# Reordering the first passes of a fused attention and MLP kernel: maxima, gate factors, weight loads and the first finished x

## The reference

```python
# attention: B=4, H=8, S=576, D=64
scores = scale * q @ k^T, causal mask
a = exp(scores - rowmax); a /= a.sum(-1) + 1e-9
local = a @ v
q_p = phi(q)                       # phi(x) = (x if x > 0 else exp(x) - 1) + 1
mem_out = (q_p @ M_prev) / (q_p . z_prev + 1e-6)
g = 1 / (1 + exp(-beta))
x = g * mem_out + (1 - g) * local  # -> 2304 tokens x 512
# MLP 1 (512 -> 2048 -> 512)
h = x @ w_in;  g = h if h >= 1 else 0 if h <= -1 else (h + 1)^2 / 4;  x = g @ w_out
# MLP 2, same sizes
h = x @ w_in2; out = max(0.01 * h, h) @ w_out2
```

## Time and profile before

| what | value |
|---|---|
| median of 3 runs | 999.5 us |
| lowest, highest run | 999.47, 1002.23 us |
| the profiled execution's own time | 999.27 us |
| its span | 997.1 us |
| mean granted TensorE clock | 0.999 |
| PE busy | 990.2 us (99%) |
| DVE, ACT, POOL busy | 447.1, 513.7, 426.6 us |

### The profile page before, as it was taken

How to read it: one execution, slowest core, us unless ns; L and a number is a source line. 1 busy time by engine, 2 the same in 40 slices (tenths; PEclk the granted TensorE clock), 3 DMA queues, 4 the chain that set the end, 5 groups by cost and what they waited for, 6 DMA issues and landing times.

```text
span 997.1 us, 16651 instructions
## 1 busy us (share of the span) xinstructions
PE 990.2 (99%) x6201; PEld 871.8 (87%) x6201; DVE 447.1 (45%) x1113; ACT 513.7 (52%) x1121; POOL 426.6 (43%) x377
## 2 busy tenths in 40 slices
PE   9999999999999999999999999999999999999998
PEld 6889899999999999999999998888888888888897
DVE  6787856676667566666422274112111111211111
ACT  7887676767676776767433474223222222322121
POOL 3588656564645546465422286222222222222222
PEclk9999999999999999999999999999999999999999
DMA  7572422333214224132110453002000200200010
GB/s 239 169 238 64 98 55 65 80 80 80 83 52 109 54 59 105 53 89 52 40 44 22 127 194 103 22 1 63 1 22 1 64 22 1 64 1 0 1 43 21
DMA packets 98432, 66.74 MB, mean 67 GB/s; under 512 B 74416, under 2 KB 87984, under 8 KB 98352
## 3 DMA queue, kind: packets, MB, share of 16 engines
q1 hardware_dynamic: 97472, 62.80, 22.8%
q10 hardware_dynamic: 880, 2.88, 0.9%
HBM read 54.54 MB, written 11.07 MB: 66 GB/s over the span
## 4 chain that ended last, share of the span: by engine, by line
PE 96%; ACT 1%; DVE 1%; issue 1%; POOL 1%; DVEq 0%; ACTq 0%; POOLq 0%
PE Hp L722 13%; PE Hp L721 13%; PE Hp L723 13%; PE Yp L745 8%; PE Yp L746 7%; PE Yp L751 7%; PE At L746 6%; PE At L745 6%; PE At L751 6%; PE At L640 5%; PE At L668 4%; PE At L564 4%; PE At L615 1%; PE At L656 1%; PE Hp L564 1%
## 5 line engine op out<-in xcount | busy, mean ns | idle before, releaser
L1371 POOL TENSOR_TENSOR Gl<-Gl_raw,Gh 128x512 fp32r<-128x512 f32 x144 | 191.9, 1332 | 434.4 <-ACT Gh L985 434.4
L721 PE MATMUL Hp<-Xh,WAh 128*128 128x256 f32 (+1 forms) x704 | 214.6, 305 | 0.0
L722 PE MATMUL Hp<-Xl,WAh 128*128 128x256 f32 (+1 forms) x704 | 212.6, 302 | 0.0
L723 PE MATMUL Hp<-Xh,WAl 128*128 128x256 f32 (+1 forms) x704 | 212.6, 302 | 0.0
L1205 DVE TENSOR_TENSOR Gl_raw<-Hp,Gl_raw 128x512 f32<-128x512 f32 x72 | 49.8, 692 | 297.5 <-ACT Gl_raw L977 297.5
L977 ACT ACTIVATE Gl_raw<-Hp 128x512 f32<-128x512 f32 x72 | 43.1, 599 | 230.3 <-PE Hp L723 230.3
L721 PEld LDWEIGHTS Hp<-Xh,WAh 128*128 128x128 f32 x704 | 134.0, 190 | 8.2 <-issue 0.4
L722 PEld LDWEIGHTS Hp<-Xl,WAh 128*128 128x128 f32 x704 | 134.1, 190 | 7.7
L985 ACT ACTIVATE Gh<-Gl_raw 128x512 fp32r<-128x512 f32 x144 | 90.9, 631 | 94.2 <-DVE Gl_raw L1205 52.4
L723 PEld LDWEIGHTS Hp<-Xh,WAl 128*128 128x128 f32 x704 | 134.0, 190 | 5.0
L745 PE MATMUL Yp<-WBh,Gh 128*128 128x512 f32 x320 | 132.5, 414 | 0.0
(11 more groups left out here) (157 smaller groups left out, 1934.8 us busy)
## 6 DMA issues: line engine op xcount, KB each, us to landing
raw<-long SPq DMA_DIRECT2D x16, 480.0 KB, 4.0
WBl_raw<-w_out SPq DMA_DIRECT2D x14, 512.0 KB, 3.9
WAl_raw<-w_in SPq DMA_DIRECT2D x13, 512.0 KB, 4.8
Vs_raw<-v_long SPq DMA_DIRECT2D x16, 320.0 KB, 3.6
yT_scratch<-xraw SPq DMA_DIRECT2D x36, 128.0 KB, 2.5
prob<-yT_scratch SPq DMA_DIRECT2D x9, 512.0 KB, 4.1
out<-prob SPq DMA_DIRECT2D x34, 128.0 KB, 2.2
raw<-short SPq DMA_DIRECT2D x11, 384.0 KB, 3.4
```

Of the source, the lines that this page charges most:

```text
L721: pe.matmul(h, WAh[:, f, j, :], xh, start=(j == 0), stop=False)
L722: pe.matmul(h, WAh[:, f, j, :], xl, start=False, stop=False)
L723: last = pe.matmul(h, WAl[:, f, j, :], xh, start=False, stop=(j == DT - 1))
L1371: gp.tensor_tensor(Gl[:, U % 2, :], act[:, U % 2, :], Gh[:, U % 2, :].bitcast(F32), ALU.subtract).then_inc(g_lo, 1)
```

## The change

Only the passes without MLP work are changed. On DVE, `factors(0)` is cut in two (`row_sums`, `inverses`), and in pass 1 slot 1's maxima stand ahead of `lay_gates` and of both halves. `inverses(1)` moves into pass 2, behind the maxima of slot 2. `row_max(1, h)` waits for the exponents of slot 0, since `negmax` is shared. On SP, `send_sums(0)`, `send_sums(1)`, `spread_factors(0)` and `spread_factors(1)` go later. On ACT, `phi_exponent(1)` goes ahead of `memory_out(0)`, the gates' exponent goes behind `exps(0, 1)`, `memory_out(1)` ahead of `plain_weights(0)`, and loads and splits of weights go later by a pass or so. On PE, `scores(n)` starts with the wide tiles and waits for the last maximum only ahead of bank 1. On POOL, the first `scale_memory` and `finish` wait for `rt_out` of 3, which is the end of `factors(2)`. Half of the split of the first output weights goes to the end of pass 5.

```diff
@@ -470,12 +470,21 @@
                 if n < OPENING - 2:
                     load_qkm(front + 2)
-                if back is not None:
+                if n == 2:
+                    send_sums(1)
+                    spread_factors(0)
+                if n > 2:
                     spread_factors(back)
                 if n >= OPENING - 2:
                     load_qkm(front + 2)
                 load_v(front + 1)
-                send_sums(front)
+                if n == 1:
+                    send_sums(0)
+                if n == 2:
+                    spread_factors(1)
+                if n > 1:
+                    send_sums(front)
                 if last is not None:
@@ -574,7 +583,8 @@
                     pe.wait_ge(k_lo, split_before(n + 1))
                 if n < OTHER_BANKS:
-                    after(pe, max_done, tiles_before(n))
+                    after(pe, max_done, tiles_before(n) - 1 if n else 0)
                 else:
@@ -583,7 +593,9 @@
                     last = memory(n)
                 if part(n) == 0:
-                    for q0, width, col, _, _ in reversed(TILES[0]):
+                    for q0, width, col, _, _ in TILES[0] if n < OTHER_BANKS else reversed(TILES[0]):
+                        if col == BANK and n < OTHER_BANKS:
+                            after(pe, max_done, tiles_before(n))
                         tile = both_heads(n, q0, (0, 0), width, (col // BANK, col // BANK), col % BANK)
@@ -683,6 +695,7 @@
                         transposes(back, 0, n)
                     after(pe, pt_lo, low_before(front - 1))
+                    after(pe, mem_out, front)
                     memory(front).then_inc(mem_done, 1)
@@ -885,14 +898,14 @@
                 if n == 0:
                     exps(0, 0)
-                    sc.wait_ge(beta_in, 16)
-                    sc.wait_ge(table_in, 1)
-                    sc.activation(gates[:, 1, :], gates[:, 0, :], ACT.Exp, scale=-1.0).then_inc(gates_exp, 1)
+                    phi_exponent(1)
+                if n == 1:
+                    memory_out(front)
                 if back is not None:
                     plain_weights(back)
-                memory_out(front)
-                if n == 1:
-                    load_second(1)
+                if n != 1:
+                    memory_out(front)
                 if n >= 3:
@@ -904,16 +917,24 @@
                     if n > 0:
                         exps(front, 0)
-                    phi_exponent(front + 1)
+                    if n == 2:
+                        split_second(0)
+                    if n > 0:
+                        phi_exponent(front + 1)
                 exps(front, 1)
                 if n == 0:
+                    sc.wait_ge(beta_in, 16)
+                    sc.wait_ge(table_in, 1)
+                    sc.activation(gates[:, 1, :], gates[:, 0, :], ACT.Exp, scale=-1.0).then_inc(gates_exp, 1)
+                    load_second(0)
+                if n == 1:
                     load_first(1)
                     split_first(0)
-                if n == 1:
+                if n == 2:
+                    load_second(1)
+                    split_first(1)
+                if n == 3:
                     load_first(2)
-                    split_second(0)
-                if n == 2:
-                    split_first(1)
                 if n == OPENING - 1:
@@ -1000,7 +1021,6 @@
             phi_exponent(0)
             load_first(0)
-            load_second(0)
             sc.wait_ge(zeroed, 3)
@@ -1032,6 +1052,9 @@
                 ve.wait_ge(s_done, n + 1)
                 after(ve, t_done, turned_before(n - 1))
+                if n == 1:
+                    ve.wait_ge(p_exp, NT[0] * (h + 1))
                 for i, (_, width, _, at, _) in enumerate(TILES[part(n)]):
@@ -1078,19 +1101,31 @@
                     ve.wait_ge(x_part, 2 * split_before(b) + h + 1)
                     ve.tensor_tensor(x, At[D * h:D * h + D, 2 + h, 0:ql], x, ALU.add).then_inc(x_sum, 1)
+            def norms(n):
+                ve.wait_ge(norm_done, n + 1)
+                after(ve, rt_out, n)
+                ve.tensor_scalar(rnr[:, 6:RN].rearrange("p (h i) -> p h i", h=2)[:, :, 0:len(NORM_TILES)],
+                                 norm_cols.rearrange("p (i h) -> p h i", h=2), 1e-6, None, ALU.add).then_inc(norm_in, 1)
             def factors(n):
+                row_sums(n)
+                inverses(n)
+            def row_sums(n):
                 ve.wait_ge(p_exp, tiles_before(n + 1))
-                after(ve, sums_sent, 16 * n)
+                after(ve, rt_out, n)
                 if n < OPENING:
-                    ve.wait_ge(norm_done, n + 1)
-                    ve.tensor_scalar(rnr[:, 6:RN].rearrange("p (h i) -> p h i", h=2)[:, :, 0:len(NORM_TILES)],
-                                     norm_cols.rearrange("p (i h) -> p h i", h=2), 1e-6, None, ALU.add).then_inc(norm_in, 1)
+                    if n > 0:
+                        norms(n)
                     ve.tensor_tensor(rnr[:, 0:6], rn[:, 0:6], rn_tiny[:, 0:6], ALU.add).then_inc(rn_sum, 1)
                     ve.wait_ge(norm_in, n + 1)
                 else:
                     ve.wait_ge(n_cut, 32 * (n - OPENING + 1))
                     after(ve, norms_sent, 16 * (n - OPENING))
                     ve.tensor_tensor(rnr[:, 0:RN], rn[:, :], rn_tiny[:, :], ALU.add).then_inc(rn_sum, 1)
+            def inverses(n):
+                after(ve, sums_sent, 16 * n)
                 ve.wait_ge(rn_sum, n + 1)
@@ -1150,6 +1185,11 @@
                 row_max(front, 0)
                 row_max(front, 1)
+                if n == 1:
+                    row_sums(0)
+                if n == 2:
+                    inverses(1)
                 if back is not None:
@@ -1158,12 +1198,18 @@
                 if front + 1 not in LEAST_ON_SCALAR:
                     least_q(front + 1)
+                if n == 1:
+                    lay_gates()
                 if back is not None:
                     plain_sum(back)
                 phi_sum(front + 1)
                 if n == 0:
-                    lay_gates()
-                factors(front)
+                    norms(0)
+                if n == 1:
+                    inverses(0)
+                    row_sums(1)
+                if n > 1:
+                    factors(front)
             def lay_gates():
@@ -1181,6 +1227,9 @@
             def split_weights(s, f):
                 ve.wait_ge(wb_hi, FT * s + f + 1)
+                if s == 0 and f == 2:
+                    ve.wait_ge(wb_lo, 2)
                 ve.tensor_tensor(WBl[:, f, :], WBraw[:, f, :], WBh[:, f, :].bitcast(F32), ALU.subtract).then_inc(wb_lo, 1)
@@ -1331,10 +1380,12 @@
                     split_first(0)
                 if n == 2:
-                    split_second(0)
+                    split_second_tile(0)
                 if last is not None:
                     if last == 0:
-                        gp.wait_ge(wb_lo, 2)
+                        gp.wait_ge(wb_lo, 1)
+                        gp.wait_ge(rt_out, 3)
                     elif n == OPENING - 2:
...
```

More of the change, by code:

```diff
@@ L1347, in opening, with split_second_tile @@
                 if n == OPENING - 1:
+                    split_second_tile(1)
                     gp.wait_ge(rt_out, OPENING)
                     split_first(2)
-            def split_second(u):
-                f = slice(2 * u, 2 * u + 2)
-                gp.wait_ge(wb_hi, 2 * u + 2)
-                gp.tensor_tensor(WBl[:, f, :].rearrange("p a m -> p (a m)"), WBraw[:, f, :].rearrange("p a m -> p (a m)"),
-                                 WBh[:, f, :].rearrange("p a m -> p (a m)").bitcast(F32), ALU.subtract).then_inc(wb_lo, 2)
+            def split_second_tile(f):
+                gp.wait_ge(wb_hi, f + 1)
+                gp.tensor_tensor(WBl[:, f, :], WBraw[:, f, :], WBh[:, f, :].bitcast(F32), ALU.subtract).then_inc(wb_lo, 1)
             def split_first(u):
```

## The result

The changed kernel takes 1003.83 us (median of 16 runs, 1001.84 to 1007.71), the kernel before 1000.19 us (16 runs, 998.34 to 1002.92). The ratio is 1.0041, 95% interval 1.0032 to 1.0050: slower by 3.6 us and above the forecast range. The profiled execution is the slowest of the 16, 1007.71 us, so its waits show more than a typical run has.

A forecast was written before the change was run, and what follows sets the result against it. PE, busy 990.2 of 997.1 us, bounds the kernel through the first MLP matmul's start. Terms -1.14, +0.7, -0.64 + 0.5, +1.4 and +0.2 make 1.0, on 999.27 giving 1000.3 us; range 998.2 to 1002.3.

The forecast's parts named there:

- The first steps: Passes 1 to 4: -1.14 us in pass 1, +0.7 in pass 2, -0.64 + 0.5 in pass 3, +1.4 in pass 4.
- The send was to hold `inverses(1)`: Pass 2, DVE: `send_sums(0)` taking 2.6 us, `sums_sent` at 18.7, `inverses(1)` waiting for it; PE waits 0.7 us.
- The term for pass 0: End of pass 0, PE: `scores(1)` may start before the last maximum, saving 0 to 0.18 us, taken as 0.16.
- x(3) follows `factors(3)` by a fixed chain, from 29.58 to the end of its split at 40.64: Ahead of the MLP: starting 1.3 us later, it ends at 41.95, so the first MLP matmul starts about 41.97.
- +0.2 (x(3)): Last term of the sum: waiting for x(3) ahead of the first MLP matmul adds 0.2 us.
- what moved had slack: Moved weight loads and splits: ACT was idle or early there, and first use of their results is behind 40.97 us.
- The bound of 4.9 us: Landing of the spread: 3.3 to 4.9 us, median 3.5; with a 4.00 send the slow bound adds 2.8 us.
- x(0) late, so ACT late: `x_done(0)` at 27.1, not 24.67, delays ACT's `split_slot(0)` and slot 3's exponents; `scores(5)` at 35.7, before 34.87.
- The send and the spread meet full DMA engines: Rival, chance 0.12: send 4.00 us and landing 4.9 put `x_done(0)` at 29.9, `scores(5)` at 38.5; 1003.1 us.
- The clock falls: Rival, chance 0.02: after PE waits in passes 2 to 4 the clock drops, adding 3 to 6 us; 1002 to 1006.
- The gain stays: Rival, chance 0.14: passes 1 and 3 become steady, nothing is late; 1.8 us gained, 997.5 us.
- no change at all: Rival: x(0) late by about what passes 1 and 3 gained; 999.0 to 999.6 us, counted in the forecast.

The follow-up runs named there:

- e2: Changed kernel, with POOL's first 128x1024 split waiting until slot 1's row sums are added; 1.0050.
- e3: Changed kernel, with SP issuing `spread_factors(0)` ahead of `send_sums(1)`; 1.0036.
- e4: Changed kernel with both the edits of e2 and e3; 1.0031, 1002.5 us.
- e6: Changed kernel, with all five first weight loads issued where the kernel before has them, splits as changed; 1.0038.
- e5: Changed kernel, with `load_first(2)` issued at the end of pass 4 instead of pass 3; 1.0045.
- e7: Changed kernel, without POOL's wait for `rt_out` of 3 ahead of x(0); 1.0043.
- e9: Changed kernel, with POOL's half split of output weights held back until x(3) is split; 1.0031.
- e13: Changed kernel, with small matmuls that compute nothing of the output put into PE's waits; 1.0038.
- e1: Kernel before, with only the new score tile order and the wait for the last maximum only ahead of bank 1; 1.0003.
- e15: Kernel before, with only POOL's wait for `rt_out` of 3 ahead of x(0); 1.0008, 1001.05 us.
- e16: Kernel before, with only the 512 KB `load_first(2)` moved from pass 1 to the end of pass 3; 1.0003.
- e8: Changed kernel with the edits of e2, e3, e6 and e7 together; 1.0023, 1002.09 us.
- e10: e8 plus the edit of e9, POOL's half split of output weights behind the split of x(3); 1.0013.
- e11: e10, with ACT splitting x(0) behind the exponents of slot 3's first head, not ahead of them; 1.0000, 999.84 us.
- e17: e11 with two buffers for `rt`, so `inverses(n)` waits for the send of slot n - 2; 0.9992, 999.45 us.
- e18: e12 with two buffers for `rt`; 1.0020, 1001.62 us.
- e12: e11, with weight loads where the change puts them and `load_first(2)` in pass 4; 1.0009, 1001.52 us.
- e14: e11, with small matmuls that compute nothing of the output in pass 2 and ahead of the first MLP matmul; 1.0009.

## Why the prediction was wrong

**The first steps held.** In the changed profile pass 1 lasted 6.22 us (6.20 forecast), the row-sum addition of `factors(2)` 0.15, and ACT stood idle 2.03 and 1.38 us ahead of `memory_out(3)` and of Xh of slot 0 ("some 2 us"). In e2's profile the whole road stands nearly where it was forecast: the wait of pass 2 is 0.67 (0.7), the start of `factors(3)` 30.74 (30.9), `scores(5)` 35.54 (35.7). Part of this was luck. The forecast had x(0) start at 24.2 because the spread lands then, and held that `rt_out` of 3 comes about 23 and doesn't bind; in e2, e3, e4 and e6 it is `rt_out` that binds, at 24.1 to 24.9, and where the landing binds (changed, e5, e7, e9, e13) x(0) starts at 24.9 to 27.9. The send was to hold `inverses(1)`: it did so for 0.17 us in e2 and for nothing in the changed profile. The term for pass 0, at most 0.18 us, was too sure: the scores of slot 0 alone take 1.3 to 2.4 us from one profile to the next (e1).

**The step that failed** is "x(3) follows `factors(3)` by a fixed chain, from 29.58 to the end of its split at 40.64", with "+0.2 (x(3))" in the sum. In e2, `factors(3)` started at 30.74 and the MLP at 44.46: 13.72 us where the forecast took 11.39 (40.97 - 29.58), 2.5 us over the 41.97 that the text gives. From `factors(3)` to the MLP it was 11.4 to 11.5 us in the profiles of before, e1 and e15, 12.1 in e16, and 12.7 to 14.8 in the eight of the changed kernel and of e2 to e5, e7, e9 and e13 (12.5 in e6). The chain isn't fixed, because `spread_factors(3)` waits for the third spread to land, and DVE's split of x(3) shares its time with POOL. From the start of `factors(3)` to the fourth spread went 3.03 us before (29.58 to 32.61), 5.54 in the changed kernel (34.20 to 39.74), 4.98 in e2 (30.74 to 35.72). With the load of 512 KB away from the third spread it was 3.15 (e5) and 3.08 (e6). The split of x(3) takes 1.02 us, and 0.42 before, beside the half split of weights moved to the end of pass 5 (46.74, 1.26 us); with that split held back it takes 0.42 again (e9). The forecast said that what moved had slack, and looked at when the results are needed; it didn't look at what the moved work runs beside. The Trainium skill ("SBUF — State Buffer", Who interferes with whom), which the forecast used for the gain alone, has the shared port pair of VectorE and GpSimd as an exclusive lock; the 0.15 and 2.36 us of the same addition agree with it. The fixed cost of about 2.0 us that the forecast quotes from the Trainium skill ("DMA: Bandwidth & Descriptors", Anatomy of one DMA) stands there for DMAs issued by GpSimd; the sends here are issued by SP, and no term of the sum used it.

**A smaller error is the landing time.** The bound of 4.9 us came from the six DMAs of the earlier trace rows with early loads. After, the median is 4.9 and the longest 6.9; with `load_first(2)` in pass 4 (e5) the longest is 4.9, with all loads early (e6) 4.0. Alone on the kernel before, the later load also lengthens it (6.4, e16), but costs nothing there, since x(2) then waits only 0.54.

**What the 3.6 us consist of.** By ratios the way back is: changed 1.0041; four edits (e8) 1.0023; five (e10) 1.0013; with ACT's order (e11) 1.0000; with the second `rt` buffer (e17) 0.9992. Only the stretch from the changed kernel to e10, 2.8 us, is clear of noise; the later steps, 1.3 and 0.8 us, overlap in their intervals. Late loads cost 2.2 us where the other waits are gone (e18 against e17), though hardly anything in the changed kernel, by ratios 0.3 (e6, 1.0038 against 1.0041). None of the five edits alone (1.0031 to 1.0050) can be told from the changed kernel. That each wait hides the next fits this, and e5 shows one case of it, where the moved load holds the fourth spread and no longer the third; as an account of the whole it is argued and not shown. The mechanism "x(0) late, so ACT late" was forecast and seen (e15).

**The clock is the second step that failed.** It had a chance of 0.02, since before every pass had 1.00. The mean clock was under 0.999 in 13 of the 16 runs of the changed kernel (median 1004.49) and at or above it in 3 (1001.91). The same split shows in e11 (9 at 999.68, 3 at 1003.84), e12 (11 at 1001.46, 1 at 1003.63), e10 (5 at 1000.30, 7 at 1002.61) and e18 (7 at 1001.19, 4 at 1003.37); all 11 runs of e17, the kernel with the shortest waits, were at or above 0.999. So about 2 us of the median go with the lower clock (1003.83 against 1001.91, the latter from 3 runs only and inside the forecast range). The 3.0 us in the changed profile and the 5.5 us at the lower level in e10's show it directly. In the seven profiles with such a fall in their first 60 us (changed, e4, e7, e9, e10, e13, e14) it came behind a PE wait of 1.66 to 3.61 us. That the waits bring the fall is still not shown: waits of 2.23 (e5), 2.48 (e16) and 2.72 us (e11) had none behind them, the last as long as e10's, and the fillers decided nothing.

**The rivals.** "The send and the spread meet full DMA engines" gave 1003.1, close to the time, for a reason that held in part: landings were longer than its 4.9, but the send hardly held `inverses(1)` (nothing in the changed profile, 0.17 us in e2, 0.57 in e9), and x(0) was done at 30.4 in the profile and about 26.9 in e2. "The clock falls" gave 1002 to 1006 and was real. "The gain stays" and "no change at all" fell. The true course was the forecast one, plus the last chain, plus the clock in most runs; my range had no room for two of them together.

## What to carry to other kernels

When a step is moved, follow it to every instruction that it will then run beside, on POOL and DVE and in the DMA queues, and not only to whoever needs its result; a chain that holds a DMA or a POOL and DVE pair is never "fixed". When a producer gets later, look first at what stands behind its consumer in that engine's queue (e15: x(0) 2.6 us later, the MLP 1.0 later). Where several small waits lie on one path, undo them together before the single ones are judged: five edits gave 2.8 us together and nothing clear one by one. Take a dozen runs and not one profile, which can be 4 us off their median, and where the runs fall into two groups by their clock, compare within a group too, because the median jumps from one group to the other.

## What the runs showed of the hardware

- An addition of 128x6 elements takes 0.15 us or 2.36 us. It was held for the whole of POOL's 128x1024 operation at starts of 15.64 against 15.62 (changed), 15.92 against 15.90 (e7) and 17.23 against 17.14 (e16). It wasn't held at 16.27 against 16.26 (e3), nor at 15.70 against 15.68 (e5), 16.70 against 16.69 (e6), 15.37 against 15.36 (e9) and 15.60 against 15.59 (e13); in these five POOL's operation took 2.40 us and not 2.35. A start difference as small as the profile can tell decides 2.2 us, which makes executions of one kernel differ.
- The spread of 160 KB over partitions landed in 3.4 to 6.9 us in the changed kernel, with late loads of 512 KB, and in 3.0 to 4.1 where the loads were issued early (e6, e17). The send of 16 KB held DVE until 3.9 us after its issue in e10 (15.50 to 19.4) with early loads.
- TensorE's granted clock was at its lower level (0.50) from 48.9 to 52.1 us in the changed profile, after waits of 0.77 and 1.66 us, and from 22 to 24 after one of 2.29. After a wait of 2.72 us it was there from 22.0 to 27.5 in e10 and stayed at 1.00 in e11.
